# Spreading in one piece, values in four pieces per pair of heads, and scores begun one half tile ahead

## The chip, the cores and the metric

The kernel runs on one core of one Trainium2 chip. The metric is the device time of one launch in microseconds (us). The engines are PE (matrix products), DVE (vector), ACT (scalar functions and copies), POOL (GpSimd) and SP, which here only starts transfers.

## The reference, cut to what matters

Four batches of eight heads, 576 positions, 64 wide; then two layers of 2304 tokens.

```python
def _attn_ref(q, k, v, tau):
    scores = q.shape[-1] ** -0.5 * np.matmul(q, k.transpose(0, 1, 3, 2))
    thresh = np.max(scores, axis=-1, keepdims=True) - tau
    scores = np.where(scores >= thresh, scores, -1000000000.0)
    attn = np.exp(scores - np.max(scores, axis=-1, keepdims=True))
    attn = attn / (np.sum(attn, axis=-1, keepdims=True) + 1e-09)
    return np.matmul(attn, v)
# x: (2304, 512) from the heads; w_in (512, 2048), w_out (2048, 512)
h = x @ w_in;  x = (h * np.tanh(softplus(h))) @ w_out       # layer 1
h = x @ w_in2; x = (h * np.clip(h + 3, 0, 6) / 6) @ w_out2  # layer 2
```

## The kernel before, in words

Attention comes first, then the two layers. Both layers split their products into blocks (seven products in place of eight) and each product into high and low parts; that code is untouched but for the rounding of late weights.

Attention takes heads in pairs. A pair has nine tiles of 128 queries (4.5 per head; the tile in the middle holds the last 64 queries of one head and of the other). Eight iterations of two pairs, 18 tiles each, make 144 tiles. I call the tile's number in its pair i (0 to 8), and a step is what an engine does for one tile.

In a step PE computes the scores of tile t in two halves, each with a high and a low part of k, into one of three pairs of PSUM banks (line 590). A half may be 256 or 320 keys wide. Then it does a piece of the previous pair's work, if one is due: the spreading of the reciprocal sums over the partitions (L626) or the products of values (L648, and L657 for the 64 keys left over, the tail). Last it turns tile t-2: for odd i and for i = 8 first the tail (L601), then the four main blocks (L606). The turned tail lies in the last 128 columns of a pair of score banks, so the second half of a tile's scores waits until ACT has copied out the tail that was there (`tail_kept`); the first half waits only for `probs_ready`.

DVE takes the maximum of tile t (L1061), weighs tile t-1 (L1045: probabilities and their sum), and computes the threshold of tile t (L1072). At i = 0 it computes totals and reciprocals of the pair that has just ended (L1077, L1079); at i = 1 and 6 it scales a part of the mixed values (L1052).

ACT, in order: the copy of the spread sums at i = 2 and 3 (L837), the turned tail (L825), the exponential (L844), the turned main blocks (L818). Behind some steps it rounds k of heads 2 and 3 (steps 3 and 5 of the 18, L802), weights for the layers in four parts (steps 15, 16, 17 and 1, L857), and in the last two iterations x (L873).

POOL splits q and k of the next heads, mixes and splits weights. Its copy of the low part of k waits for ACT's rounding. SP's order of transfers is the same before and after; only counts that it waits for differ.

Each engine's order is the written one: an instruction that waits holds up all behind it on its engine.

The numbers of the pieces are in two tables, which say at which i which groups of keys are multiplied (0 to 3 main, 4 tail), for the lower and the upper part of the queries:

```python
part0 = {4: (0,), 5: (1, 2), 6: (3, 4)}
part1 = {7: (0, 1), 8: (2,), 0: (3,), 1: (4,)}
```

## Time and profile before

| | us |
|---|---|
| time of three runs | 1042.05, 1040.82, 1039.70 |
| median | 1040.82 |
| the profiled execution, time | 1039.75 |
| the profiled execution, span in the trace | 1037.8 |
| PE busy | 1017.1 (98%) |
| DVE busy | 864.2 (83%) |
| ACT busy | 639.7 (62%) |
| POOL busy | 548.1 (53%) |

The time is that of the launch, the span what the engines' records cover; 1.95 us lie around it. The granted TensorE clock is 1.0 of full speed (2.4 GHz) in every stretch. Matmuls overlap in the records, and their ends are modelled: the time that a matmul takes up is the distance from its start to the next one's, not its duration. A product of plain fp32 operands has two records for one instruction, so eight records of L626 are four instructions.

### The profile page before, as it was taken

Reading aid. Unit: us, or ns where it says so; the run is one execution under the profiler, and the core shown is the slowest. Engines: PE = TensorE matmul, PEld = TensorE weight load, DVE = VectorE, ACT = ScalarE, POOL = GpSimd, SP = SyncE. Lnnn points to the kernel's source line nnn. Section 1 sums busy time; section 2 is a strip of 40 time slices with the busy share of each in tenths; the row PEclk is TensorE's granted clock in tenths of the full one; section 3 lists DMA queues with packets and bytes.
Section 4 is the critical chain, followed back from the end, with each engine's and each line's share of the span. In section 5 each row is a group of like instructions: output and inputs, shape, how many; then the busy total and the mean of one; then the engine's idle time right before and its main releaser. Section 6 shows DMA issues by size and latency. Waiting matters only on the chain.

```text
span 1037.8 us, 20190 instructions
## 1 busy us (share of the span) xinstructions
PE 1017.1 (98%) x6984; PEld 928.0 (89%) x6984; DVE 864.2 (83%) x1712; ACT 639.7 (62%) x1209; POOL 548.1 (53%) x578
## 2 busy tenths in 40 slices
PE   5999999999999999999999999999999999999998
PEld 4777777777778999999999999999999999999998
DVE  7888888888875999789997999867996779967884
ACT  5767777778874566455665566555564556555543
POOL 6898898899974830278005750178003850078200
PEclk9999999999999999999999999999999999999999
DMA  6375466467434889589894889643795447753674
GB/s 184 113 218 178 141 214 193 142 205 211 137 113 167 279 298 366 179 269 312 285 392 147 273 303 344 227 147 130 254 310 178 145 170 279 258 172 108 223 244 162
DMA packets 137571, 224.92 MB, mean 217 GB/s; under 512 B 9728, under 2 KB 77824, under 8 KB 137472
## 3 DMA queue, kind: packets, MB, share of 16 engines
q1 hardware_dynamic: 137472, 223.65, 64.8%
q8 instruction: 56, 0.92, 0.4%
q14 instruction: 43, 0.35, 0.1%
HBM read 173.02 MB, written 50.59 MB: 215 GB/s over the span
## 4 chain that ended last, share of the span: by engine, by line
PE 72%; DVE 13%; ACT 6%; issue 5%; DMA 1%; DVEq 0%; ACTq 0%
PE banks L590 7%; PE banks L648 7%; PE banks L606 6%; PE banks L760 6%; PE banks L759 6%; PE banks L758 6%; PE banks L766 5%; PE banks L767 5%; PE banks L768 5%; PE banks L723 5%; PE banks L725 5%; PE banks L724 5%; ACT relu L921 3%; PE banks L657 2%; DVE first_kept L1121 2%
## 5 line engine op out<-in xcount | busy, mean ns | idle before, releaser
L1386 POOL TENSOR_TENSOR ring<-raw,ring 128x256 fp32r<-128x256 f32 x336 | 280.6, 871 | 385.0 <-ACT ring L886 385.0
L723 PE MATMUL banks<-x_high,ring 128*128 128x384 f32 x672 | 228.0, 339 | 3.9 <-ACT first_kept L898 1.7
L725 PE MATMUL banks<-x_high,ring 128*128 128x384 f32 x672 | 225.0, 335 | 0.0
L724 PE MATMUL banks<-x_low,ring 128*128 128x384 f32 x672 | 224.9, 335 | 0.0
L759 PE MATMUL banks<-ring,g_high 128*128 128x256 f32 x504 | 142.6, 283 | 0.0
L760 PE MATMUL banks<-ring,g_low 128*128 128x256 f32 x504 | 142.6, 283 | 0.0
L758 PE MATMUL banks<-ring,g_high 128*128 128x256 f32 x504 | 142.6, 283 | 0.0
L1061 DVE TENSOR_REDUCE neg_max<-banks 128x1 f32<-128x576 f32 x144 | 107.8, 749 | 41.0 <-PE banks L590 38.8
L723 PEld LDWEIGHTS banks<-x_high,ring 128*128 128x128 f32 x672 | 126.1, 188 | 14.2 <-issue 9.4
L724 PEld LDWEIGHTS banks<-x_low,ring 128*128 128x128 f32 x672 | 126.2, 188 | 0.0
L725 PEld LDWEIGHTS banks<-x_high,ring 128*128 128x128 f32 x672 | 126.2, 188 | 0.0
L844 ACT ACTIVATE exps<-banks,neg_max 128x576 f32<-128x576 f32 x144 | 108.1, 751 | 21.8 <-DVE neg_max L1061 21.0
L1045 DVE SCALAR_TENSOR_TENSOR probs<-banks,thresh,exps 128x576 f32<-128x576 f32 x144 | 116.4, 808 | 0.2 <-ACT exps L844 0.2
L766 PE MATMUL banks<-g_high,ring 128*128 128x384 f32 x336 | 112.3, 334 | 0.3 <-DMA ring<-w_out_mix 0.3
L768 PE MATMUL banks<-g_low,ring 128*128 128x384 f32 x336 | 112.2, 334 | 0.0
L767 PE MATMUL banks<-g_high,ring 128*128 128x384 f32 x336 | 112.2, 334 | 0.0
L590 PE MATMUL banks<-k_high,q_stack 128*128 128x256 f32 (+1 forms) x320 | 102.0, 335 | 7.6 <-DVE k_low L1036 7.6
L760 PEld LDWEIGHTS banks<-ring,g_low 128*128 128x128 f32 x504 | 96.7, 192 | 0.0
L759 PEld LDWEIGHTS banks<-ring,g_high 128*128 128x128 f32 x504 | 96.7, 192 | 0.0
L758 PEld LDWEIGHTS banks<-ring,g_high 128*128 128x128 f32 x504 | 96.7, 192 | 0.0
L606 PE MATMUL banks<-ident,probs 128*128 128x128 f32 x576 | 89.7, 278 | 3.8 <-ACT probsT L818 2.9
L936 ACT CAST g_high<-g_rest 128x384 fp32r<-128x384 f32 x120 | 61.6, 514 | 49.3 <-PE banks L760 26.7
(104 smaller groups left out, 2245.4 us busy)
## 6 DMA issues: line engine op xcount, KB each, us to landing
ring<-w_out_mix SPq DMA_DIRECT2D x168, 512.0 KB, 5.1
raw<-w_in_mix SPq DMA_DIRECT2D x48, 896.0 KB, 5.8
w_in_mix<-prep_in SPq DMA_DIRECT2D x18, 896.0 KB, 4.9
w_out_mix<-prep_high SPq DMA_DIRECT2D x16, 896.0 KB, 4.4
w_out_mix<-prep_low SPq DMA_DIRECT2D x16, 896.0 KB, 6.5
q_raw<-qT SPq DMA_DIRECT2D x64, 144.0 KB, 2.9
k_raw<-kT SPq DMA_DIRECT2D x64, 144.0 KB, 3.0
prep_in<-w_in SPq DMA_DIRECT2D x64, 128.0 KB, 3.1
```

Of the source, the lines that this page charges most:

```text
L590: mm = nc.tensor.matmul(bank_pair(s)[:, begin:begin + last - first], lhs, rhs[:, first:last], start=(n == 0), stop=(n == len(products) - 1))
L606: mm = nc.tensor.transpose(turned[:, P * j:P * j + P], own[:, first + P * j:first + P * j + P], ident[:, :])
L723: nc.tensor.matmul(dst, w[:, 0, cols], high, start=(t == 0 and m < 4), stop=False, skip_group_check=True)
L724: nc.tensor.matmul(dst, w[:, 0, cols], low, start=False, stop=False, skip_group_check=True)
L725: mm = nc.tensor.matmul(dst, w[:, 1, cols], high, start=False, stop=(t == KH - 1), skip_group_check=True)
L758: nc.tensor.matmul(to, high[:, rows], w[:, 0, :], start=begin and t % 2 == 0, stop=False, skip_group_check=True)
L759: nc.tensor.matmul(to, high[:, rows], w[:, 1, :], start=False, stop=False, skip_group_check=True)
L760: mm = nc.tensor.matmul(to, low[:, rows], w[:, 0, :], start=False, stop=end, skip_group_check=True)
L766: nc.tensor.matmul(dst[:, d, :], w[:, 0, cols], high, start=begin, stop=False, skip_group_check=True)
L767: nc.tensor.matmul(dst[:, d, :], w[:, 1, cols], high, start=False, stop=False, skip_group_check=True)
L768: mm = nc.tensor.matmul(dst[:, d, :], w[:, 0, cols], low, start=False, stop=end, skip_group_check=True)
L1386: nc.gpsimd.tensor_tensor(ring_slot(slot)[:, 1, :], raw[q % 2][:, m, :], f32(ring_slot(slot)[:, 0, :]), ALU.subtract).then_inc(w_low_ready, 1)
```

## The change

Five things are changed.

First, the pieces. The spreading is done at i = 2 in one piece (its 64 tail columns go to a score bank, the 512 main ones to bank 7), and ACT copies it in two instructions one behind the other. Values come at i = 4 (key groups 0, 1, 2), 6 (3, 4), 8 (0, 1, 2 of the upper part) and 0 (3, 4). So steps 1, 3, 5 and 7 have no piece.

Second, the order on PE. In an odd step PE computes both halves of tile t and the first half of tile t+1, then turns tile t-2; in the even step that follows it starts with the second half. Which tiles have their tail turned in one transpose with their neighbour is numbered anew; the number of transposes stays.

Third, DVE: odd steps take the maximum and the threshold only, even steps weigh tile t-1 and then tile t at once. At i = 0 the totals come between the maximum and the threshold of tile 0, and only tile 0 is left to weigh. The scaling of the lower part moves from i = 6 to i = 7.

Fourth, ACT: in even steps the exponential comes first. k is rounded at steps 4 and 6 in place of 3 and 5. Weights are rounded in three parts at steps 17, 0 and 1, and those that are prepared during the layers in two parts in place of four, on ACT and on DVE.

Fifth, behind the last tile the remaining pieces of attention and the first seven products of the layer are written out in a new order with fewer changes between them.

The core of the diff:

```diff
     def tail_first(i):
-        return i % 2 == 1
-    def turns_tail(i):
-        return tail_first(i) or i == PAIR_TILES - 1
+        return i % 2 == 1 or i == PAIR_TILES - 1
     def tail_rows(i):
-        return UPPER if turns_tail(i) else LOWER
+        return UPPER if i % 2 == 1 else LOWER
...
+        SPREAD_AT = 2
+        MIX0_AT = {4: (0, 1, 2), 6: (3, 4)}
+        MIX1_AT = {8: (0, 1, 2), 0: (3, 4)}
...
+        spread_main = banks[:, 7, 0:MAIN * P]
+        def spread_tail(pair):
+            bank = 1 if pair < PAIRS - 1 else 5
+            return banks[:, bank, BANK - P:BANK - P + TAIL]
...
-        PREP_PARTS = (slice(0, 2), slice(2, 4), slice(4, 6), slice(6, MIXES))
+        PREP_PARTS = (slice(0, 3), slice(3, 5), slice(5, MIXES))
+        LATE_PARTS = (slice(0, 4), slice(4, MIXES))
+        def parts_of(unit):
+            return PREP_PARTS if unit < QUADS - 1 else LATE_PARTS
...
+                if half == 0:
+                    if i in (0, MAIN):
+                        pe.wait_ge(q_low_ready[2 * p + i // MAIN], it + 1)
+                        pe.wait_ge(k_low_ready[2 * p + i // MAIN], it + 1)
+                    after(pe, probs_ready, t - 2)
+                else:
+                    after(pe, tail_kept, tails_turned(max(t - 2, 0)))
+                    if i == SPREAD_AT + 1:
+                        after(pe, spread_kept, 2 * (it * PAIRS_IT + p) - 1)
...
-            part0 = {4: (0,), 5: (1, 2), 6: (3, 4)}
-            part1 = {7: (0, 1), 8: (2,), 0: (3,), 1: (4,)}
-            def attention_step(it, s, ahead=True):
+            def attention_step(it, s):
                 t, p, i = it * TILES_IT + s, s // PAIR_TILES, s % PAIR_TILES
-                first = isinstance(it, int) and it == 0
-                if ahead:
-                    score_tile(it, s)
                 pair, b = it * PAIRS_IT + p - 1, (p + 1) % 2
-                if not first or p == 1:
-                    if i in (2, 3):
-                        spread_sums(pair, b, i - 2)
-                    if i in part0:
-                        mix(it, pair, b, 0, part0[i])
-                    if i in (7, 8):
-                        mix(it, pair, b, 1, part1[i])
-                if not first and i in (0, 1):
-                    mix(it, pair - 1, 1 - b, 1, part1[i])
-                if (not first or s >= 2) and (ahead or s < 2):
+                if even(i):
+                    if i == 0:
+                        score_half(it, s, 0)
+                    score_half(it, s, 1)
+                    if i == SPREAD_AT and pair >= 0:
+                        spread_sums(pair, b, t)
+                    if i in MIX0_AT and pair >= 0:
+                        mix(it, pair, b, 0, MIX0_AT[i])
+                    if i == 8 and pair >= 0:
+                        mix(it, pair, b, 1, MIX1_AT[i])
+                    if i == 0 and pair >= 1:
+                        mix(it, pair - 1, 1 - b, 1, MIX1_AT[i])
+                else:
+                    score_half(it, s, 0)
+                    score_half(it, s, 1)
+                    score_half(it, s + 1, 0)
...
+            last, b = PAIRS - 1, (PAIRS - 1) % 2
+            end = ITS * TILES_IT
+            pe.wait_ge(tail_kept, tails_turned(end - 2))
+            up(0, 0, A11_B11)
+            up(0, 0, S1_T1)
+            mix(ITS, last - 1, 1 - b, 1, MIX1_AT[0])
+            turn(end - 2, TILES_IT - 2)
+            pe.wait_ge(tail_kept, tails_turned(end - 1))
+            up(0, 0, S2_T2)
+            up(0, 0, S3_T3)
+            turn(end - 1, TILES_IT - 1)
+            pe.wait_ge(tail_kept, tails_turned(end))
+            spread_sums(last, b, end + 1)
+            up(0, 0, A12_B21)
+            mix(ITS, last, b, 0, range(MAIN + 1))
+            up(0, 0, S4_B22)
+            mix(ITS, last, b, 1, range(MAIN + 1))
+            up(0, 0, A22_T4)
...
+            def keep_spread(pair):
+                act.wait_ge(spread_ready, pair + 1)
+                nc.scalar.copy(spread[:, MAIN * P:SEQ], spread_tail(pair)).then_inc(spread_kept, 1)
+                nc.scalar.copy(spread[:, 0:MAIN * P], spread_main).then_inc(spread_kept, 1)
+            def take_exp(t, s):
+                act.wait_ge(max_ready, t + 1)
+                after(act, probs_ready, t - 1)
+                nc.scalar.activation(exps[:, s % 2, :], scores_of(s), ACT.Exp,
+                                     bias=neg_max[:, s % 3:s % 3 + 1], scale=1.0).then_inc(exp_ready, 1)
+            rounds = {4: 2, 6: 3}
+            def attention_step(it, s):
                 t, p, i = it * TILES_IT + s, s // PAIR_TILES, s % PAIR_TILES
-                first = isinstance(it, int) and it == 0
-                if i in (2, 3) and (not first or p == 1):
-                    u, pair = i - 2, it * PAIRS_IT + p - 1
-                    act.wait_ge(spread_ready, 2 * pair + u + 1)
-                    nc.scalar.copy(spread[:, PART_AT[u]:PART_AT[u + 1]], mixed[u]).then_inc(spread_kept, 1)
-                if (not first or s >= 2) and (ahead or s < 2):
-                    keep_tail(t - 2, (s - 2) % TILES_IT)
-                if ahead:
-                    act.wait_ge(max_ready, t + 1)
-                    after(act, probs_ready, t - 1)
-                    nc.scalar.activation(exps[:, s % 2, :], scores_of(s), ACT.Exp,
-                                         bias=neg_max[:, s % 3:s % 3 + 1], scale=1.0).then_inc(exp_ready, 1)
-                if (not first or s >= 2) and (ahead or s < 2):
-                    keep_main(t - 2, (s - 2) % TILES_IT, it * PAIRS_IT + (s - 2) // PAIR_TILES)
-                if ahead and s in rounds:
+                pair, pair2 = it * PAIRS_IT + p - 1, it * PAIRS_IT + (s - 2) // PAIR_TILES
+                if even(i):
+                    take_exp(t, s)
+                    if i == SPREAD_AT and pair >= 0:
+                        keep_spread(pair)
+                    if t >= 2:
+                        keep_tail(t - 2, (s - 2) % TILES_IT)
+                        keep_main(t - 2, (s - 2) % TILES_IT, pair2)
+                else:
+                    if t >= 2:
+                        keep_tail(t - 2, (s - 2) % TILES_IT)
+                    take_exp(t, s)
+                    if t >= 2:
+                        keep_main(t - 2, (s - 2) % TILES_IT, pair2)
+                if s in rounds:
...
-                    if s in (15, 16, 17) and it < ITS - 1:
-                        round_prep(0, it, s - 15)
-                    if s == 1 and it > 0:
-                        round_prep(0, it - 1, 3)
+                    if s == 17 and it < ITS - 1:
+                        round_prep(0, it, 0)
+                    if s < 2 and it > 0:
+                        round_prep(0, it - 1, 1 + s)
...
-                after(dve, main_turned, t - 1)
+                after(dve, main_turned, t - 1 if i == 1 else t - 2)
...
                                         mixed[u], spread[:, PART_AT[u]:PART_AT[u + 1]], ALU.mult).then_inc(x_ready, 1)
-            def attention_step(it, s, ahead=True):
+            def take_recips(pair, b):
+                dve.wait_ge(probs_ready, (pair + 1) * PAIR_TILES)
+                nc.vector.tensor_scalar(totals[:, b, :], sums[:, b, :], 1e-9, None, ALU.add).then_inc(totals_ready, 1)
+                dve.wait_ge(totals_ready, pair + 1)
+                nc.vector.reciprocal(recips[:, b, :], totals[:, b, :]).then_inc(recips_ready, 1)
+            def attention_step(it, s):
                 t, p, i = it * TILES_IT + s, s // PAIR_TILES, s % PAIR_TILES
-                first = isinstance(it, int) and it == 0
-                if ahead:
-                    dve.wait_ge(scores_ready, t + 1)
-                    nc.vector.tensor_reduce(neg_max[:, s % 3:s % 3 + 1], scores_of(s), AX_X, ALU.max,
-                                            negate=True).then_inc(max_ready, 1)
                 pair, b = it * PAIRS_IT + p - 1, (p + 1) % 2
-                if i == 6 and (not first or p == 1):
+                if i == 7 and pair >= 0:
                     scale_mixed(pair, 0)
-                if i == 1 and not first:
+                if i == 1 and pair >= 1:
                     scale_mixed(pair - 1, 1)
-                if (not first or s >= 1) and (ahead or s < 1):
-                    weigh(t - 1, (s - 1) % TILES_IT)
-                if ahead:
-                    dve.wait_ge(max_ready, t + 1)
-                    nc.vector.tensor_scalar(thresh[:, s % 3:s % 3 + 1], neg_max[:, s % 3:s % 3 + 1], -1.0, tau_abs[:, :],
-                                            ALU.mult, ALU.subtract).then_inc(thresh_ready, 1)
-                if i == 0 and (not first or p == 1) and (ahead or s == 0):
-                    dve.wait_ge(probs_ready, (pair + 1) * PAIR_TILES)
-                    nc.vector.tensor_scalar(totals[:, b, :], sums[:, b, :], 1e-9, None, ALU.add).then_inc(totals_ready, 1)
-                    dve.wait_ge(totals_ready, pair + 1)
-                    nc.vector.reciprocal(recips[:, b, :], totals[:, b, :]).then_inc(recips_ready, 1)
+                dve.wait_ge(scores_ready, t + 1)
+                nc.vector.tensor_reduce(neg_max[:, s % 3:s % 3 + 1], scores_of(s), AX_X, ALU.max,
+                                        negate=True).then_inc(max_ready, 1)
+                if i == 0 and pair >= 0:
+                    take_recips(pair, b)
+                elif even(i) and i > 0:
+                    weigh(t - 1, s - 1)
+                dve.wait_ge(max_ready, t + 1)
+                nc.vector.tensor_scalar(thresh[:, s % 3:s % 3 + 1], neg_max[:, s % 3:s % 3 + 1], -1.0, tau_abs[:, :],
+                                        ALU.mult, ALU.subtract).then_inc(thresh_ready, 1)
+                if even(i):
+                    weigh(t, s)
...
```

How the orders differ, at three places. PE, step 5 of a first pair and the start of step 6, before (`k_high_85`, `k_low_86`: head 1; L648: values of the previous pair; L601 and L606: the turn of tile 3, L601 its tail):

```order
L590 MATMUL banks<-k_high_85,q_stack_84 128x320 [waits probs_ready]
L590 MATMUL banks<-k_low_86,q_stack_84 128x320
L590 MATMUL banks<-k_high_85,q_stack_84 128x256 [waits tail_kept]
L590 MATMUL banks<-k_low_86,q_stack_84 128x256
L648 MATMUL banks<-probsT_80,values 64x256 x4
L601 MATMUL banks<-ident,probs 128x128 [waits probs_ready]
L606 MATMUL banks<-ident,probs 128x128 [waits main_kept]
L606 MATMUL banks<-ident,probs 128x128 x3
L590 MATMUL banks<-k_high_85,q_stack_84 128x256 [waits probs_ready]
L590 MATMUL banks<-k_low_86,q_stack_84 128x256
L590 MATMUL banks<-k_high_85,q_stack_84 128x320 [waits tail_kept]
```

and now (L610 scores, L622 and L627 the turn):

```order
L610 MATMUL banks<-k_high_78,q_stack_77 128x320 [waits probs_ready]
L610 MATMUL banks<-k_low_79,q_stack_77 128x320
L610 MATMUL banks<-k_high_78,q_stack_77 128x256 [waits tail_kept]
L610 MATMUL banks<-k_low_79,q_stack_77 128x256
L610 MATMUL banks<-k_high_78,q_stack_77 128x256 [waits probs_ready]
L610 MATMUL banks<-k_low_79,q_stack_77 128x256
L622 MATMUL banks<-ident,probs 128x128 [waits probs_ready]
L627 MATMUL banks<-ident,probs 128x128 [waits main_kept]
L627 MATMUL banks<-ident,probs 128x128 x3
L610 MATMUL banks<-k_high_78,q_stack_77 128x320 [waits tail_kept]
L610 MATMUL banks<-k_low_79,q_stack_77 128x320
```

The piece between scores and turn is gone, the first half of tile 6 (its 256 keys) has moved up in front of the turn, and what stands right behind the turn is now the half that waits for `tail_kept`, for the very tail whose transpose stands four transposes ahead of it.

ACT, steps 0, 1 and the start of 2, before (L857: rounding of weights):

```order
L825 COPY tailT<-banks 128x128 [waits tail_turned]
L844 ACTIVATE exps<-banks,neg_max 128x576 [waits probs_ready,max_ready]
L818 COPY probsT_89<-banks 128x4x128 [waits main_turned]
L825 COPY tailT<-banks 128x128 [waits tail_turned]
L844 ACTIVATE exps<-banks,neg_max 128x576 [waits probs_ready,max_ready]
L818 COPY probsT_89<-banks 128x4x128 [waits main_turned]
L857 CAST prep_high<-prep_out 128x256 [waits prep_out_stored,prep_out_mixed]
L837 COPY spread<-banks 128x256 [waits spread_ready]
L844 ACTIVATE exps<-banks,neg_max 128x576 [waits probs_ready,max_ready]
```

and now (L901: rounding of weights; L862, L863: copies of the spread sums):

```order
L870 ACTIVATE exps<-banks,neg_max 128x576 [waits probs_ready,max_ready]
L856 COPY tailT<-banks 128x128 [waits tail_turned]
L849 COPY probsT_89<-banks 128x4x128 [waits main_turned]
L901 CAST prep_high<-prep_out 128x512 [waits prep_out_stored,prep_out_mixed]
L856 COPY tailT<-banks 128x128 [waits tail_turned]
L870 ACTIVATE exps<-banks,neg_max 128x576 [waits probs_ready,max_ready]
L849 COPY probsT_89<-banks 128x4x128 [waits main_turned]
L901 CAST prep_high<-prep_out 128x512 [waits prep_out_stored,prep_out_mixed]
L870 ACTIVATE exps<-banks,neg_max 128x576 [waits probs_ready,max_ready]
```

Two roundings (of 512 each) stand here now where one of 256 stood, one in front of the tail copy of step 1 and one in front of the exponential of step 2; those of steps 15 and 16 are gone.

DVE, two steps, before and now (L1045 and L1090 weigh, L1061 and L1116 take the maximum, L1072 and L1123 compute the threshold):

```order
L1061 TENSOR_REDUCE neg_max<-banks 128x1 [waits scores_ready]
L1045 SCALAR_TENSOR_TENSOR probs,sums<-banks,thresh,exps 128x576 [waits main_turned,thresh_ready,exp_ready]
L1072 TENSOR_SCALAR thresh<-neg_max,tau_abs 128x1 [waits max_ready]
L1061 TENSOR_REDUCE neg_max<-banks 128x1 [waits scores_ready]
L1045 SCALAR_TENSOR_TENSOR probs,sums<-banks,thresh,exps 128x576 [waits main_turned,thresh_ready,exp_ready]
L1072 TENSOR_SCALAR thresh<-neg_max,tau_abs 128x1 [waits max_ready]
```

```order
L1116 TENSOR_REDUCE neg_max<-banks 128x1 [waits scores_ready]
L1123 TENSOR_SCALAR thresh<-neg_max,tau_abs 128x1 [waits max_ready]
L1116 TENSOR_REDUCE neg_max<-banks 128x1 [waits scores_ready]
L1090 SCALAR_TENSOR_TENSOR probs,sums<-banks,thresh,exps 128x576 [waits main_turned,thresh_ready,exp_ready]
L1123 TENSOR_SCALAR thresh<-neg_max,tau_abs 128x1 [waits max_ready]
L1090 SCALAR_TENSOR_TENSOR probs,sums<-banks,thresh,exps 128x576 [waits main_turned,thresh_ready,exp_ready]
```

The second weighing follows the maximum of its own tile with one weighing and one threshold between them; before, a whole step lay between.

## Rows read from the trace of the kernel before

**Rows 1.** Windows: attention, layers. Busy PE, PEld, DVE, ACT, POOL; clock, DMA share, GB/s.
```profile
24.50:304.50 280.00, 278.48 (x2273) 206.38 (x2271) 235.85 (x596) 211.87 (x422) 249.85 (x222) 1.00 0.56 174
324.70:1037.80 713.10, 706.30 (x4496) 696.62 (x4494) 604.50 (x1054) 404.57 (x747) 270.88 (x322) 1.00 0.70 238
```

**Rows 2.** Waits in 100 to 200 us: who waited for whom, total, times, longest.
```profile
ACT tailT L825 <- PE banks L601: 17.3, 21, 1.4
```

**Rows 3.** PE timeline, first pair. Start, duration, engine, line, names, shape, count.
```profile
15.10 0.31 PE L590 MATMUL banks<-k_low,q_stack 128*128 128x320 f32 x1
15.25 0.60 PE L606 MATMUL banks<-ident,probs 128*128 128x128 f32 x4
15.60 0.39 PE L590 MATMUL banks<-k_high,q_stack 128*128 128x320 f32 x1
```

**Rows 4.** PE timeline, last tile of a pair with a values piece.
```profile
171.19 0.31 PE L590 MATMUL banks<-k_low,q_stack 128*128 128x320 f32 x1
171.43 0.76 PE L648 MATMUL banks<-probsT,values 128*64 128x320 f32 x4
172.12 0.66 PE L606 MATMUL banks<-ident,probs 128*128 128x128 f32 x4
172.53 0.36 PE L590 MATMUL banks<-k_high,q_stack 128*128 128x256 f32 x1
```

**Rows 5.** PE timeline, end of attention (bracket: idle before, releaser).
```profile
305.58 0.41 PE L723 MATMUL banks<-x_high,ring 128*128 128x384 f32 x1 [0.81 <-issue]
...
308.54 0.33 PE L601 MATMUL banks<-ident,probs 128*128 128x128 f32 x1
...
309.23 0.44 PE L723 MATMUL banks<-x_high,ring 128*128 128x384 f32 x1
...
314.58 0.77 PE L626 MATMUL banks<-ident,recips 128*64 128x128 f32 x12 [0.70 <-ACT spread L837]
...
320.16 1.83 PE L648 MATMUL banks<-probsT,values 128*64 128x320 f32 x12
```

**Rows 6.** ACT timeline, the copy of the tail between two of those.
```profile
308.91 0.27 ACT L825 COPY tailT<-banks 128x128 f32<-128x128 f32 x1 [0.86 <-PE banks L601]
```

**Rows 7.** PE timeline, first spreading piece of a pair.
```profile
177.36 0.66 PE L626 MATMUL banks<-ident,recips 128*64 128x128 f32 x8
178.20 0.63 PE L606 MATMUL banks<-ident,probs 128*128 128x128 f32 x4 [0.18 <-ACT probsT L818]
```

**Rows 8.** ACT timeline, main copy, rounding of k, exponential.
```profile
166.74 0.59 ACT L818 COPY probsT<-banks 128x512 f32<-128x512 f32 x1
167.20 0.69 ACT L802 CAST k_high<-k_raw 128x576 fp32r<-128x576 f32 x1
167.78 0.76 ACT L844 ACTIVATE exps<-banks,neg_max 128x576 f32<-128x576 f32 x1
```

**Rows 9.** ACT timeline, a rounding of x in the last iteration.
```profile
273.92 0.85 ACT L873 CAST x_high<-x_mix 128x768 fp32r<-128x768 f32 x1
```

**Rows 10.** DVE timeline, totals of a pair, three pairs in a row.
```profile
137.28 1.06 DVE L1077 TENSOR_SCALAR totals<-sums 128x9 f32<-128x9 f32 x1
...
156.17 0.41 DVE L1077 TENSOR_SCALAR totals<-sums 128x9 f32<-128x9 f32 x1
...
174.89 1.06 DVE L1077 TENSOR_SCALAR totals<-sums 128x9 f32<-128x9 f32 x1
```

**Rows 11.** POOL timeline, the operation beside the first of them.
```profile
137.16 1.15 POOL L1327 TENSOR_TENSOR q_stack<-q_raw,q_scale 128x576 fp32r<-128x576 f32 x1
```

**Rows 12.** DVE timeline, a reduce that waits, then two weighings.
```profile
162.97 0.76 DVE L1061 TENSOR_REDUCE neg_max<-banks 128x1 f32<-128x576 f32 x1 [0.84 <-PE banks L590]
...
178.64 0.81 DVE L1045 SCALAR_TENSOR_TENSOR probs<-banks,thresh,exps 128x576 f32<-128x576 f32 x1
...
180.17 0.81 DVE L1045 SCALAR_TENSOR_TENSOR probs<-banks,thresh,exps 128x576 f32<-128x576 f32 x1
```

**Rows 13.** ACT timeline, the exponential behind the reduce of 162.97 us.
```profile
163.77 0.75 ACT L844 ACTIVATE exps<-banks,neg_max 128x576 f32<-128x576 f32 x1 [0.26 <-DVE neg_max L1061]
```

97 lines of the change are left out of this document (42 added, 55 removed).

## The prediction, made before the changed kernel ran

> **What bounds the kernel now.** I read the page first. PE is busy 98% of the span, but ends of matmuls are modelled, so that share proves little. I then cut the span by stages [rows 1]. From 24.5 to 304.5 us, attention, PE shows 278.5 of 280 us, DVE 236, ACT 212, POOL 250; the clock is 1.00. From 324.7 us on, the layers, PE shows 706.3 of 713.1 us. The change touches attention almost alone, so the question is what sets the 280 us.
>
> The waits give it: ACT stood 17.3 us in 100 for the turned tail [rows 2], and DVE stands for scores (0.84 us before the maximum of 162.97 us, [rows 12]), while DVE needs 1.53 us from one weighing to the next where nothing holds it (178.64 to 180.17 us, [rows 12]): 13.8 us for nine tiles. The totals of three successive pairs start at 137.28, 156.17 and 174.89 us [rows 10]: two pairs take 37.61 us, so a pair takes 18.8. PE sets it: DVE and ACT stand for PE in most steps, PE hardly ever for them. What PE saves counts in full, and what makes PE wait costs in full.
>
> Next I looked at how PE's time is spent when it changes the kind of its products. In the first pair no piece of older work is due: the last score product starts at 15.10, the first transpose at 15.25, the next scores at 15.60 us [rows 3]. 0.15 us is what a product of 320 columns takes, so this change costs nothing, and four transposes take 0.35 us. With a piece of values between, the last score product starts at 171.19, the piece at 171.43 (0.24: 0.09 more), the transposes at 172.12 and the next scores at 172.53 us (0.41: 0.06 more) [rows 4]. The four records of the piece take 0.69 us. Twelve such records last 1.83 and four 0.76 us [rows 5, 4], so four more cost 0.54 us, and 0.15 us of the 0.69 is fixed. A piece costs 0.09 + 0.15 + 0.06 = 0.30 us beside its products.
>
> The Trainium skill says it too ("TensorEngine Tiling (Array Packing)", Key Properties): changing the tiling mode drains the engine. The pieces write 64 columns of the array (128*64 in the rows), scores and transposes 128. The trace agrees, at 0.30 us for the way there and back. What the rule alone would make of the change is a rival below.
>
> **The change, part by part.** The sum is made against the profiled execution, 1039.75 us (span 1037.8 and 1.95 around it); it lies 1.07 us under the median of the three runs, 1040.82, and I add the sum to the median.
>
> (a) *Fewer pieces.* Before, each of nine steps has one, now five (i = 0, 2, 4, 6, 8). The products are the same ones. Four fewer, at 0.30 us, are -1.20 us in each of the 15 pairs in which pieces are done: -18.0 us. In the steps with a tail, where the 0.06 us may not show, it may be 0.23 us: -13.8 us.
>
> (b) *The tail's hand-over.* In an odd step PE now turns tail and main blocks of tile t-2 and then starts the second half of tile t+1, which waits until ACT has copied that tail. Before, the first half stood between and hid it. The end of attention shows the price: tail transpose 308.54, ACT's copy 308.91, the waiting product 309.23 us [rows 5, 6], 0.69 us from transpose to product, with 0.16 us of it a wait by the weight loads. Without the wait PE would need 0.09 (one transpose, a quarter of 0.35) + 0.35 = 0.44 us. So each hand-over costs 0.25 us; if the first transpose still takes 0.17 as at the end, 0.17 us, and then (a) is the smaller one. All four odd steps have a tail: +1.00 us a pair, +15.0 us in 15; bounds +10.2 and, if ACT is busy at that moment, more (d, f). Queued behind the waiting half are the piece and the turn of the even step; DVE's maximum waits for it.
>
> (c) *The old wait at i = 2.* The first spreading piece has eight records from 177.36 us, and the transposes start at 178.20, of which 0.18 us is a wait for ACT's main copy [rows 7]; in the other pair of an iteration I see none with that label. I take 0.13 us a pair as gone, -2.0 us (0 to -2.7). Nothing is late next there: the totals and sums are ready two steps earlier.
>
> So (a) to (c) are -5.0 us: the large saving is handed back almost whole by (b).
>
> (d) *ACT's roundings.* After a turn ACT makes the main copy, then at steps 4 and 6 the rounding of k, then the next tail copy. Copy at 166.74, rounding 167.20, next at 167.78 us [rows 8]: 1.04 us, and 0.3 us before it (as between the tail's transpose and its copy, 0.37) make 1.34. Meanwhile PE does six score products (0.86 us by the distances of rows 3: about 0.13 each and 0.08 for the first) and its tail transpose; its copy could start 0.37 later, at 1.23. So each costs 0.1 us. The weights' parts in steps 0 and 1 each hold up something: the second, in front of the exponential of tile 2 and so of the spread sums' copy, by about 0.2 us. Together 0.4 us an iteration, in 7: +2.8 us. Lower end 0; upper end the whole of one rounding (0.69) and as much for a weights' part, 1.4 an iteration: +9.8. POOL gets the rounded k some 2.5 us later in an iteration and has had waits of that size for it, so it costs nothing until that grows.
>
> (e) *Totals.* They now stand between the maximum of tile 0 and its weighing. They last 1.06 or 0.41 us [rows 10]: the one at 137.28 ends at 138.34, and POOL's operation beside it runs from 137.16 to 138.31 us [rows 11]. The weighing must wait anyway for the exponential: maximum at 162.97, exponential at 163.77, 0.75 long [rows 12, 13], so about 1.58 us from the maximum's start; the other work fits in while the totals take up to 0.6. Excess 0.46 us in one pair of two, half of it reaching PE: +0.2 us an iteration, +1.4 us. Bounds: 0, and 1.15 us (the POOL operation) in each of 15 pairs if all reached PE, +17.
>
> The Trainium skill ("SBUF — State Buffer", Who interferes with whom) says that a tensor_scalar of DVE may take the port pair shared with GpSimd and that the second to ask is blocked until the first is done. The trace agrees (both ends within 0.03 us); by the rule the price would be 0 to one POOL operation in each pair, with the new phase unknown, which is what the bounds above say.
>
> (f) *x in the last two iterations.* Roundings of x, 0.85 us long [rows 9], follow steps 2, 4, 6 of the last iteration and step 10 of the one before. Behind a k rounding that is already late, one costs nearly its full length: 0.7 + 0.7 us, 0.5 at step 2, 0.3 before: +2.2 us (0 to +3.4).
>
> (g) *The end.* Seven pieces become four, -0.9 us; the wait of 0.70 us between the two spreading pieces at 314.58 [rows 5] is gone; one more hand-over shows, +0.16; the first product of the layer waited 0.81 us for its weights [rows 5] and will wait about 0.15 less, as the piece of step 8 is longer. -1.6 us (-2.4 to 0: the single spreading also waits for two copies, behind which the values stand).
>
> (h) *The start.* Tile 1's maximum now waits for tile 0's weighing: one maximum, 0.76 us, at most, made up in the pair that has no pieces: +0.3 us. The late roundings in two parts save two starts each on DVE and ACT, nine times, in a stage where PE is full [rows 1]: -0.3 us (-2 to +0.5, the upper if DVE waits for ACT's longer first part).
>
> Sum: -5.0 + 2.8 + 1.4 + 2.2 - 1.6 + 0.3 - 0.3 = -0.2 us. Forecast: no change, 1040.7 us, where 0.2% (2.1 us) is about what a measurement can tell from none.
>
> **The rivals.**
>
> *ACT and DVE cannot keep the chain between them (slower).* PE now has ACT's tail copy in its path four times a pair, and behind each turn ACT has main copy, rounding and tail copy in a row. It decides when the copy starts later than 0.37 us after its transpose: every 0.1 us there, in four steps and 15 pairs, is 6 us. With (d) at 1.0 us an iteration (+4.2 more than the sum), and (e) at 0.4 (+1.4 more): 1040.6 + 5.6 = 1046.2 us. For it: ACT has no slack at steps 4 and 6 by my count. Against: it was idle 17.3 us in 100 [rows 2].
>
> *The side costs are covered (faster).* If (d), (e) and (f) fall where something else waits, 6.4 us of the sum go: 1034.3 us. For it: in even steps the piece of values leaves ACT and DVE over 1 us. Against: PE is the bound, so there is little else to hide behind.
>
> *The tail is no hand-over at all (much faster).* (a), (c) and (g) stay and (b) is nothing: 1040.8 - 18.0 - 2.0 - 1.6 + 6.4 = 1025.6 us. That needs ACT's copy to be there 0.44 us after the transpose; the rows show 0.69 [rows 5, 6]. It is also what the Trainium skill's rule on modes ("TensorEngine Tiling (Array Packing)", Key Properties) would give if nothing else counted.
>
> *It doesn't do what it says: DVE becomes the bound.* In a pair of steps the two weighings are tied to the second maximum: about 1.3 us from maximum to maximum (PE's pace) and 2.4 from there to the next maximum, 3.7 four times, 2.7 at i = 0 and 0.8 of scaling: 18.3 us a pair, against PE's 18.5. So near that pair times of 18.8 may stay as they are: 1041 us, the forecast's time for another reason.
>
> **How the numbers follow.** Forecast case, with the last rival, 0.40, of which four fifths lie within 2.1 us. Slower case 0.27. Faster case 0.28. Much faster 0.05. Its own range is 1037 to 1044; as cases of both signs hold more than half, the stated one reaches into both: 1033 (the faster case with (b) a little cheap) to 1047 (the slower one), which leaves out the much faster case and the ends of (e). Faster by over 0.2%: 0.28 + 0.05 + 0.03 = 0.36. Within: 0.33. Slower: 0.27 + 0.04 = 0.31.
>
> **What would show it.** (a) From the last score product to the first transpose of a step without a piece: 0.15 us or less. (b) From a tail transpose in an odd step to the second half of the next scores: 0.69 us, and PE or its loads waiting for the tail copy about 60 times. Pairs of 18.4 us where ACT rounds nothing, 18.8 to 19.0 where it does. (d) The tail copy at steps 5 and 7 of a first pair starts 0.1 us later than in a second pair. (e) Totals whose end is that of a POOL operation. (g) No wait of 0.70 us for the copy of spread sums at the end. I am wrong if the half behind the turn doesn't wait, or if a pair takes over 19 us in the middle of attention.

## The result, and the profile after

The changed kernel takes 1048.55 us (median of 4 runs, 1048.01 to 1050.06), the one before 1041.14 on the same chip (4 runs); the ratio is 1.0074 (95% interval 1.0059 to 1.0089). It is slower by some 7.4 us. The forecast was no change, 1040.7 us, with 1033 to 1047 as its range; the measured time lies 1.5 us above it.

The windows of the profile after, as in [rows 1]: attention from the same start, in a window 20 us longer, then the layers from their second quad on (a quad is one of the groups in which a layer's upward products are done, seven products each; busy time of PE, its weight loads, DVE, ACT, POOL; clock, DMA share, GB/s).

```profile
24.50:324.50 300.00, 282.98 (x2293) 217.59 (x2293) 244.72 (x606) 223.42 (x422) 252.16 (x219) 0.98 0.53 163
340.40:1044.90 704.50, 702.01 (x4496) 697.28 (x4494) 597.23 (x1037) 402.69 (x729) 272.81 (x322) 1.00 0.70 240
```

Two things moved, in opposite directions. The second quad starts at 340.4 us where it started at 324.7: attention and its end cost 15.7 us more. From there to the end of the last product it is 702.7 us, where it was 709.7 (1043.1 - 340.4 and 1034.4 - 324.7): 7 us less. Together +8.7 us, the difference of the spans. In attention PE is busy for 283 of 300 us, where it was for 278.5 of 280 [rows 1].

What took its time is in the waits of 24.5 to 304.5 us (who waited for whom: us, times, longest; PEld, the weight loads, and PE often wait for the same thing at once, so their lines aren't added).

```profile
POOL k_low L1387 <- ACT k_high L833: 33.1, 7, 7.7
ACT tailT L856 <- PE banks L622: 13.6, 48, 0.5
PEld banks L664 <- DMA values_tail<-v: 12.6, 6, 3.9
PE banks L664 <- DMA values_tail<-v: 11.0, 6, 3.7
PEld banks L610 <- ACT tailT L856: 10.3, 31, 1.4
PE banks L610 <- ACT tailT L856: 2.9, 4, 1.1
```

The hand-over that I had forecast is there (L610 for the tail), but in front of it stands a wait that no line of the prediction names: PE waits for a pair's values six times, 11.0 us. All six waits are in the step of tile 4 in the first pair of an iteration. The PE timeline in the fourth iteration (start, duration, engine, line, names, shape, count, idle before):

```profile
170.03 0.31 PE L610 MATMUL banks<-k_high,q_stack 128*128 128x320 f32 x1
170.18 0.31 PE L610 MATMUL banks<-k_low,q_stack 128*128 128x320 f32 x1
173.25 2.83 PE L664 MATMUL banks<-probsT,values 128*64 128x256 f32 x12 [2.76 <-DMA values_tail<-v]
176.01 1.12 PE L627 MATMUL banks<-ident,probs 128*128 128x128 f32 x4
176.78 0.61 PE L610 MATMUL banks<-k_high,q_stack 128*128 128x320 f32 x1
```

Twelve products of values last 2.83 us here, and 1.51 us after one of the shorter waits; the transposes last 1.12 and 0.66. The clock tells why (windows with the granted clock third from the right: the stretch of low clock, and 4.4 us ahead of it).

```profile
172.40:179.20 6.80, 5.95 (x27) 4.43 (x28) 1.63 (x4) 1.59 (x4) 0.74 (x1) 0.50 0.11 36
168.00:172.40 4.40, 2.44 (x17) 1.87 (x15) 3.49 (x9) 3.23 (x7) 2.66 (x3) 0.99 0.58 156
```

The clock fell to 0.50 (1.2 GHz) at 172.4 us, in the wait, and stayed there 6.8 us. At 93.8, 0.6 us after the longest wait had ended, it did so for 3.4 us. An estimate: of these 10.2 us the first 0.85 are still part of the wait, and half of the other 9.35 is 4.7 us of lost time; 11.0 + 4.7 = 15.7 us, as much as attention lost.

Who was late? First POOL, then SP's issues (L430 is k_raw of head 3, L440 to L442 the values of the odd pair), and ACT behind PE's wait:

```profile
165.59 1.41 POOL L1387 TENSOR_TENSOR k_low<-k_raw,k_high 128x576 fp32r<-128x576 f32 x1
...
178.46 1.41 POOL L1387 TENSOR_TENSOR k_low<-k_raw,k_high 128x576 fp32r<-128x576 f32 x1 [7.65 <-ACT k_high L833]
```

```profile
167.02 1.10 SPq L430 DMA_DIRECT2D k_raw<-kT  x2
168.17 1.11 SPq L440 DMA_DIRECT2D values<-v  x2
169.32 0.48 SPq L441 DMA_DIRECT2D values_tail<-v  x1
169.84 0.60 SPq L442 DMA_DIRECT2D values_tail<-v  x1
```

```profile
177.16 0.59 ACT L849 COPY probsT<-banks 128x512 f32<-128x512 f32 x1 [5.10 <-PE banks L627]
177.65 0.67 ACT L833 CAST k_high<-k_raw 128x576 fp32r<-128x576 f32 x1
```

It is a ring. SP sends k_raw of head 3 when POOL has done k_low of head 1 (167.0 us), and the values stand behind it in SP's order; they land at about 173.2, 3.4 us after the last of them is issued, and PE could have used them at 170.4. PE's wait holds up its turn, so ACT's copy, so the rounding of k, which the change put behind this very step (177.65); POOL has stood 7.65 us for it, and is late with the next k_low of head 1 an iteration on. In the kernel before the same issue of the last values came at 159.40 us and PE's piece at 162.87, 3.5 us later: there was no slack to give away, and I had not looked.

What was forecast within a pair is there too. An odd step (PE timeline; L622 turns the tail, L610 of 147.21 is the half that waits for ACT's copy of it):

```profile
146.47 0.28 PE L610 MATMUL banks<-k_low,q_stack 128*128 128x256 f32 x1
146.58 0.27 PE L622 MATMUL banks<-ident,probs 128*128 128x128 f32 x1
146.69 0.63 PE L627 MATMUL banks<-ident,probs 128*128 128x128 f32 x4
147.21 0.41 PE L610 MATMUL banks<-k_high,q_stack 128*128 128x320 f32 x1
```

The turn follows the scores by 0.11 us (no piece between, as in [rows 3]) and the half waits 0.17 us: 0.63 from tail to product, where 0.11 + 0.35 would do. The second pair of an iteration takes 18.25 us (from the maximum of its tile 0 to that of the next pair's), where it was 18.89. I call it the odd pair, and the first one, in which ACT rounds k, the even pair; that one was 18.71. In the odd steps 1, 5 and 7 of an even pair the same distance from tail to product is mostly 0.75 to 0.81 us.

### The profile page after: what moved, and what is told of

Same layout as the page of the kernel before. It is cut to its first block, busy times and chain, and to the rows that moved or that the text cites. A ratio compares the mean times of both kernels' runs of the same rounds, so it can differ in the third digit from the quotient of the medians.

```text
span 1046.5 us, 20128 instructions
## 1 busy us (share of the span) xinstructions
PE 1012.6 (97%) x6984; PEld 937.2 (90%) x6984; DVE 861.9 (82%) x1694; ACT 645.3 (62%) x1184; POOL 548.7 (52%) x571
## 4 chain that ended last, share of the span: by engine, by line
PE 60%; POOL 13%; DVE 6%; ACT 5%; issue 5%; DMA 3%; SPq 3%; DVEq 0%; POOLq 0%; ACTq 0%
PE banks L741 7%; PE banks L743 7%; PE banks L742 7%; PE banks L778 6%; PE banks L777 6%; PE banks L776 6%; PE banks L785 6%; PE banks L784 6%; PE banks L786 6%; ACT relu L965 3%; POOL prep_low L1410 2%; PE banks L664 2%; POOL q_stack L1379 2%; POOL k_low L1387 2%; POOL prep_in L1396 2%
## 5 line engine op out<-in xcount | busy, mean ns | idle before, releaser
L1116 DVE TENSOR_REDUCE neg_max<-banks 128x1 f32<-128x576 f32 x144 | 108.6, 754 | 41.0 <-PE banks L610 40.4
L1090 DVE SCALAR_TENSOR_TENSOR probs<-banks,thresh,exps 128x576 f32<-128x576 f32 x144 | 117.1, 813 | 14.5 <-ACT exps L870 10.5
L610 PE MATMUL banks<-k_high,q_stack 128*128 128x320 f32 (+1 forms) x320 | 105.4, 345 | 14.2 <-DVE k_low L1080 7.9
L849 ACT COPY probsT<-banks 128x512 f32<-128x512 f32 x144 | 84.6, 588 | 32.9 <-PE banks L627 31.1
L627 PE MATMUL banks<-ident,probs 128*128 128x128 f32 x576 | 92.5, 284 | 3.9 <-ACT probsT L849 3.2
```

What stands on the lines that cost most here:

```text
L1090: nc.vector.scalar_tensor_tensor(out=probs_of(t), in0=scores_of(s), scalar=thresh[:, s % 3:s % 3 + 1], in1=exps[:, s % 2, :], op0=ALU.is_g ...
L1116: nc.vector.tensor_reduce(neg_max[:, s % 3:s % 3 + 1], scores_of(s), AX_X, ALU.max, negate=True).then_inc(max_ready, 1)
```

## The experiments

The first four runs: the ring, and the layers. Ratios are to the kernel before, with their 95% interval; it took 1041.56, 1040.61 and 1040.94 us beside the three groups of runs, which were made on three chips, so small differences between runs are safer by the ratios.

**Values earlier.**

```
                 store_prep_in(0, it - 1)
+                if it > 1:
+                    load_values(it - 1, 1)
                 load_head(it, 3)
-                if it > 1:
-                    load_values(it - 1, 1)
```

> The changed kernel, with the values of the odd pair put in front of head 3 in SyncE's order instead of behind it. Theory (the values come late because their transfer stands behind k_raw of head 3, which waits for GpSimd's k_low of head 1, and GpSimd has been made late by the moved rounding of k): the six waits of 3.7 us for values and values_tail go, and with them the low clock behind each. The iterations, of 38.6 to 42.4 us now, come to two pairs of 18.2 to 18.4 us, and the time to 1024 to 1031 us. Rival (transfers are late whatever their order, since the shorter iteration is less than GpSimd's and SyncE's work for it): the wait moves to the q or k of a head, and the time stays within 1042 to 1049. Rival (the hand-over of the tail to ScalarE is what costs): no more than 2 us change.

1034.58 us, 0.9932 (0.9920 to 0.9944): 14 us less than the changed kernel. No wait for values is left, and the clock is 1.00. The last values of the odd pair are now issued at 154.92 us, and PE's piece follows the scores at once:

```profile
154.92 0.61 SPq L442 DMA_DIRECT2D values_tail<-v  x1
```

```profile
164.51 0.31 PE L610 MATMUL banks<-k_low,q_stack 128*128 128x320 f32 x1
164.75 1.52 PE L664 MATMUL banks<-probsT,values 128*64 128x256 f32 x12
```

The place of the values' transfers in SP's order is worth the whole loss. The time stayed 3.6 us over the top of what I had expected: an iteration takes 37.2 to 37.7 us, and the last two 38.4 and 40.2 (the last one up to the first product of the layers; 37.6 and 38.2 in the kernel before).

**k at 3 and 5.**

```
-            rounds = {4: 2, 6: 3}
+            rounds = {3: 2, 5: 3}
```

> The changed kernel, with ScalarE's rounding of k back behind steps 3 and 5. Theory (the late rounding starts the ring ScalarE, GpSimd, SyncE, values, TensorE): GpSimd is done some 2.5 us sooner, the waits for the values shrink from 3.7 us to 1 us or less, and the time comes to 1028 to 1038 us. Rival (the values come late because the pairs have become shorter, not because k is rounded later): the waits stay near 3.7 us, and the time within 1045 to 1049. In either case a k cast now stands in an odd step, where GpSimd gets it sooner and the tail's hand-over may grow by 0.5 us at two steps of 18.

1033.82 us, 0.9928 (0.9916 to 0.9940). One wait for the values is left, 0.6 us. So the ring can be cut at either place.

**The late k alone, in the kernel before.** The same line, the other way round: `rounds = {4: 2, 6: 3}`.

> The kernel before, with only ScalarE's rounding of k moved from behind steps 3 and 5 to behind steps 4 and 6. Theory (the values had no slack, and this move alone makes them late): a wait for values_tail appears on TensorE, some 2 us at the middle of most iterations, and the time is 1045 to 1056 us. Rival (with pairs of 18.8 us there is room for the move): 1040 to 1042 us.

1047.95 us, 1.0064 (1.0051 to 1.0078): this line alone makes the kernel before slower by 6.4 us. The waits of its attention:

```profile
POOL k_low L1339 <- ACT k_high L802: 23.0, 7, 5.5
ACT prep_high L857 <- POOL prep_out L1356: 10.8, 6, 2.1
PEld banks L648 <- DMA values_tail<-v: 3.7, 6, 1.4
PE banks L590 <- ACT tailT L825: 3.5, 6, 0.8
PE banks L648 <- DMA values_tail<-v: 1.9, 4, 1.1
```

An iteration takes 38.2 to 38.8 us instead of 37.6. POOL is late for the rounded k here too, but it reaches PE on two paths. The values are one, 1.9 us. The larger is another, 3.5 us: POOL's mixed weights (`prep_out`) come late, ACT stands for them in front of their rounding, and PE for the tail that ACT copies behind it (ACT, then PE; in the kernel before ACT's waits for `prep_out` are 1.4 us and PE has none for the tail):

```profile
155.65 0.62 ACT L857 CAST prep_high<-prep_out 128x512 fp32r<-128x512 f32 x1 [1.83 <-POOL prep_out L1356]
```

```profile
156.49 0.42 PE L590 MATMUL banks<-k_high,q_stack 128*128 128x320 f32 x1 [0.61 <-ACT tailT L825]
```

So my theory of this run had the time right and only part of the cause; the same edit together with earlier values, which would tell the two paths apart, was not run. The changed kernel has moved these roundings to other steps and shows no such wait of ACT. The values' waits are shorter here (1.1 at most) and the clock stays up; in the changed kernel the loss is twice as large. The rival, that shorter pairs alone made the values late, falls with k at 3 and 5.

**The late rounding alone, in the kernel before.** Two parts for the units of the layers, four as ever in attention:

```
+        LATE_PARTS = (slice(0, 4), slice(4, MIXES))
-                mixes = PREP_PARTS[n]
+                mixes = parts_of(unit)[n]
```

> The kernel before, with only the late rounding in two pieces in place of four (attention stage as before). The layers of the changed kernel are 7 us shorter in the traces. Theory (the two pieces give all of it): 1034 to 1036 us, attention unchanged at 324.7 us. Rival (the two pieces give the 0.3 us of the sum in the prediction, and the 7 us come from another part of the change or from the clock): 1040 to 1041.5 us.

1036.06 us, 0.9943 (0.9928 to 0.9958): 5.5 us less, for an edit that I had put at 0.3. Attention was not unchanged in this trace: its last exponential starts at 308.0 us, before at 304.6, though nothing in that stage's work was edited; in the control below it starts at 304.4. No cause is shown for these 3.4 us. From the last exponential to the end of the span it is 726.1 us, before 733.2: 7.1 us less.

**The late rounding undone, in the changed kernel.** `LATE_PARTS` as four slices.

> The changed kernel with only the late rounding put back to four pieces. If the late rounding gives in the changed kernel what it gives in the kernel before (5.5 us by the medians of e3_before_two_late, 7 us by the traces): 1054 to 1056 us. Rival (in the changed kernel the layers are shorter for another reason): 1048 to 1050 us.

1056.52 us, 1.0153 (1.0139 to 1.0167), 8 us more than the changed kernel (0.79% by the ratios), a little over the first theory. Both ways round, the two parts are worth 5.5 to 8 us by the times, and 7.1 and 7.2 us by the distance from the last exponential to the end (731.9 us here, 724.7 in the changed kernel). The groups of DVE's low parts, in the layers of the kernel before and then of the changed one (busy us, mean ns; idle before):

```profile
L1200 DVE TENSOR_TENSOR prep_low<-prep_out,prep_high 128x512 fp32r<-128x512 f32 x27 | 26.6, 1036 | 0.0
L1200 DVE TENSOR_TENSOR prep_low<-prep_out,prep_high 128x256 fp32r<-128x256 f32 x9 | 6.4, 715 | 0.0
```

```profile
L1248 DVE TENSOR_TENSOR prep_low<-prep_out,prep_high 128x1024 fp32r<-128x1024 f32 x9 | 12.7, 1417 | 1.2 <-ACT prep_high L901 1.2
L1248 DVE TENSOR_TENSOR prep_low<-prep_out,prep_high 128x768 fp32r<-128x768 f32 x9 | 11.8, 1310 | 0.0
```

18 pieces less save 8.5 us of DVE for the same columns, 0.47 us for each. The traces show when a piece has this price: when POOL runs beside it. The four pieces of a unit in the kernel before, first with POOL busy all the time, then with POOL idle (no POOL record from 381.0 to 383.7 us):

```profile
353.15 5.38 POOL L1386 TENSOR_TENSOR ring<-raw,ring 128x256 fp32r<-128x256 f32 x5
353.59 4.34 DVE L1200 TENSOR_TENSOR prep_low<-prep_out,prep_high 128x512 fp32r<-128x512 f32 x4
381.24 2.23 DVE L1200 TENSOR_TENSOR prep_low<-prep_out,prep_high 128x512 fp32r<-128x512 f32 x4
```

With two pieces it is 2.68 and 3.17 us beside POOL, 2.09 without it (at 369.82, 346.32 and 395.85 us of the changed kernel's trace). POOL makes the low parts of the weights that PE waits for. The waits of PE and of its weight loads in the layers, before:

```profile
PEld banks L723 <- issue: 7.7, 22, 0.8
PEld banks L723 <- POOL ring L1386: 2.8, 4, 0.9
PE banks L723 <- ACT first_kept L898: 1.7, 3, 0.6
PE banks L723 <- DVE first_kept L1121: 0.9, 3, 0.5
```

and after:

```profile
PEld banks L741 <- issue: 3.8, 12, 0.5
PE banks L741 <- DVE first_kept L1169: 0.6, 3, 0.2
```

The lines of PEld and PE overlap (the loads' wait of 0.85 us that ends at 359.43 and PE's of 0.56 at 359.46 are one). PEld's alone are 10.5 us before and 3.8 after, 6.7 less, about what the layers gained. They follow the edit in both kernels: 3.5 us with the two parts in the kernel before, 10.6 with the four in the changed one. Busy, PE shows 706.3 of 713.1 us before [rows 1]; these waits were in that "full" stage. How DVE's pieces reach the weight loads is not shown link by link: most of the waits have no releaser in the profile ("issue").

**One late part.** `LATE_PARTS = (slice(0, MIXES),)`, with both mends of the ring (as the next kernel).

> As e6_both, with the late rounding of the layers in one piece instead of two. Theory (each late piece on VectorE costs some 0.8 us at its start, by 8.7 us for eight of four parts and 5.9 us for four of two, and two pieces have already taken away TensorE's waits for the weights' low parts): within 1 us of e6_both. Rival (what counts is VectorE's time, wait or no wait): nine pieces fewer at 0.8 us on VectorE, some 3 to 5 us less. Rival (the first piece is now so long that it holds up ScalarE's gates): 2 to 5 us more.

1034.08 us, 0.9929 (0.9916 to 0.9943), against 1033.66 and 0.9934 with two parts: no change. From the last exponential to the end it is 724.6 us, with two parts 724.8, and the weight loads' waits are 3.6 us. DVE has 5.3 us less to do (19.2 against 24.5 us in these pieces), and it gives nothing: what counted was PE's waits, and two parts have taken those that can be taken this way.

**Both mends**, and as its control the kernel before with two late parts and the values earlier.

> The changed kernel with both mends: the values of the odd pair in front of head 3 in SyncE's order, and k rounded behind steps 3 and 5. Theory (each mend alone removes the same wait, and what is left is other): no wait for values, iterations of 37.2 to 37.4 us as with each alone, and 1032.5 to 1034.5 us. Rival (the two remove different losses: with the values earlier the odd pairs took 18.25 us, with k earlier the even pairs 18.8 us, and together an iteration takes 37.05 us): 1030.5 to 1032 us.

1033.66 us, 0.9934 (0.9922 to 0.9945): the first theory, one wait removed by either mend. Iterations take 37.3 to 37.4 us, and the last two 37.6 and 38.0.

> The kernel before with the late rounding in two pieces and the values of the odd pair in front of head 3: the control. Theory (with pairs of 18.8 us the values arrive just in time, so an earlier order has nothing to give): as e3_before_two_late, 1034 to 1037 us. Rival (an earlier transfer also frees GpSimd or SyncE for what follows): 1031 to 1033 us. The distance to e6_both is what the change's attention part is worth without the late values.

1032.97 us, 0.9932 (0.9919 to 0.9944). That is the top of the rival's range, but its interval overlaps both that of the late parts alone and that of both mends, so whether the earlier values give anything here stays open. So the change's attention part, freed of the ring, is worth nothing that can be measured, as the sum of the prediction had it. Both mends put k back behind steps 3 and 5; the run with the values earlier alone keeps it where the change put it, and lies 1.6 us above this control by the times and level with it by the ratios (0.9932 both).

**A sixth piece.** Both mends, and key 2 in a piece of its own behind the turn of tile 4's step.

```
-        MIX0_AT = {4: (0, 1, 2), 6: (3, 4)}
+        MIX0_AT = {4: (0, 1), 6: (3, 4)}
...
+                if i == 4 and pair >= 0:
+                    mix(it, pair, b, 0, (2,))
```

> As e6_both, but the values' piece of step 4 is cut in two, with the turn between (keys 0 and 1 before it, key 2 behind it): one more piece of 64-column products in each pair, the same products in all. It measures the price of a piece. By the prediction's 0.30 us: 15 pairs, 4.5 us more than e6_both. By the rows of the changed kernel (last score to mix 0.09 us, mix to turn 0.07, the turn behind it 0.05): about 0.2 us, 3 us more. Rival (TensorE has time to spare in this step, and a piece is paid by waits): 0 to 1 us more.

1040.02 us, 6.4 us more: 0.42 us in each of 15 pairs, above the 0.30 of the prediction. The piece itself costs 0.34 us in every pair (from the maximum of tile 4 to that of tile 5 2.91 us, with both mends alone 2.57). An odd pair wins as much back by shorter totals. Of the even ones three take 19.1 us, 0.35 more than with both mends, and three 20.0: these three are the ones whose totals last 1.36 to 1.38 us. So the rest of the 6.4 us is totals that fell beside other operations of POOL, and not the price of a piece.

**No half ahead.** Both mends; both halves of a tile's scores stand together in every step.

```
-                    if i == 0:
-                        score_half(it, s, 0)
+                    score_half(it, s, 0)
                     score_half(it, s, 1)
...
-                    score_half(it, s + 1, 0)
```

> As e6_both, but TensorE no longer begins the next tile's scores ahead of a turn: both halves of a tile stand together in every step, and the even step's first half covers the hand-over of the tail. If the hand-over is a cost of the size in the prediction (0.25 us at four places in a pair), it goes: 15 pairs by 1.0 us, 1019 to 1023 us by that price, 1029 to 1032 by the 0.15 us that the rows of the changed kernel show in every second pair. Rival (the half in front of the turn lets VectorE start its maximum 0.46 us sooner, and VectorE waits for scores as often as TensorE for the tail): it costs more than it gives, 1034 to 1040 us.

1042.09 us, 8.4 us more, above the rival's range. The hand-over is gone, and PE waits at the turns instead (attention of this run, then of both mends):

```profile
PEld banks L627 <- ACT probsT L846: 20.2, 58, 0.5
PE banks L627 <- ACT probsT L846: 7.7, 27, 1.2
```

```profile
PEld banks L610 <- ACT tailT L856: 5.7, 20, 1.0
PE banks L627 <- ACT probsT L849: 3.2, 6, 1.5
```

There is one bank for turned blocks; the half in front of the turn covers ACT's main copy out of it. DVE's waits for scores, my rival's reason, rose only from 19.6 to 23.6 us: its direction was right, its mechanism at most a part. Part of the 8.4 us is again the totals, which last 1.02 to 1.08 us in most even pairs here: such pairs take 19.7 to 19.8 us, the two with short ones 19.2, with both mends 18.8.

**Totals.** Once without the instruction, once made by ACT; both with both mends.

```
-                nc.vector.tensor_scalar(totals[:, b, :], sums[:, b, :], 1e-9, None, ALU.add).then_inc(totals_ready, 1)
-                dve.wait_ge(totals_ready, pair + 1)
-                nc.vector.reciprocal(recips[:, b, :], totals[:, b, :]).then_inc(recips_ready, 1)
+                nc.vector.reciprocal(recips[:, b, :], sums[:, b, :]).then_inc(recips_ready, 1)
```

> As e6_both, but the instruction that adds 1e-9 to a pair's sums is left out and the reciprocal reads the sums themselves (the 1e-9 is missing from the result). In e6_both this instruction of 9 columns lasts 0.99 us at 212.82 us, until GpSimd's operation beside it ends, and stands in front of the first weighing; an odd pair takes 18.57 us with it, 18.25 where it happened to be short. Theory (it holds up TensorE through the first weighing): 0.3 to 0.5 us in each of 15 pairs, 5 to 8 us less than e6_both. Rival (the wait only moves to the reciprocal, which asks for the same port): no change. Rival (VectorE has time to spare there): no change, and the reciprocal short.

1030.93 us, 0.9902 (0.9888 to 0.9916): 2.7 us less, half of the 5 to 8 that I had expected. Only the odd pairs in the middle have the long totals, and they go from 18.57 to 18.17 us. The reciprocal doesn't take it over (DVE, attention):

```profile
L1104 DVE RECIPROCAL recips<-sums 128x9 f32<-128x9 f32 x15 | 3.1, 204 | 0.0
```

And on ACT, ahead of the first exponential of a pair:

```
+                nc.scalar.activation(totals[:, b, :], sums[:, b, :], ACT.Identity, bias=tiny[:, :],
+                                     scale=1.0).then_inc(totals_ready, 1)
```

> As e6_both, with the pair's totals (sums plus 1e-9) made by ScalarE ahead of the first exponential, where it waits 0.8 us for VectorE, instead of by VectorE. If the totals on VectorE cost 0.3 to 0.5 us a pair: 1026 to 1029 us. If VectorE now stands for ScalarE's totals, or the port wait moves to the reciprocal: 1032 to 1036 us.

1032.32 us, 0.9919 (0.9906 to 0.9933). 1.3 us under both mends, and the intervals overlap: inconclusive by the times. The trace says more: an iteration takes 37.0 us, as without the totals (36.95), where it takes 37.3 to 37.4 with both mends, and 0.9 us of this are lost again in the first pair, which has a stretch of low clock in this execution (18.06 us, with both mends 17.12). It is the fastest that computes everything, with the control 0.7 us behind and not distinguishable from it.

## Why the prediction was wrong, point by point

The step that failed is the last sentence of (d): "POOL gets the rounded k some 2.5 us later in an iteration and has had waits of that size for it, so it costs nothing until that grows". A wait on an engine that has slack was taken for a wait that nothing hangs on. What hung on it in the changed kernel was SP's queue: k_raw of head 3 waits for POOL's k_low of head 1, and the values stand behind it. Measured: 14 to 15 us by either mend, the waits themselves and the low clock behind two of them. In the kernel before the same line alone costs 6.4 us, there by the values and, more of it, by POOL's late weights. The mechanism was absent from sum, bounds and rivals alike.

(h), the late rounding in two parts, was mis-sized: -0.3 (-2 at best), measured -5.5 and -8. I reasoned that in a stage where PE is full nothing on DVE can matter; the waits of that stage were never read. The share of busy time hid 10.5 us of waits of the weight loads.

The rest of the sum, +0.1 us in the forecast, came out near it: +0.7 us (both mends against their control, each known to some 1.5 us), in part because errors cancelled, which is luck:

- (a) The pieces. From one record's start to the next, in an odd pair, what leads into the pieces of values and sums or stands there in their place (1.67 us, before 2.03), and the pieces with their exits (6.92, before 7.60 without the wait of (c)), take 1.04 us less than before; forecast -1.20, the smaller bound -0.92. The sixth piece costs 0.34 by itself.
- (b) The hand-over: 0.63 us from tail to product in odd pairs, 0.17 over the 0.46 of a turn that doesn't wait. I took 0.25 and had 0.17 as bound: (a) and (b) were both too large, and their errors partly cancelled. PE's loads wait for the tail copy 31 times, not 60.
- (c) The old wait stood in the odd pairs only (0.19 us, in front of the turn at i = 2) and is gone: -1.4 us in all, where I had taken 0.13 us for every pair; where the totals are long, 0.3 to 0.4 us takes its place.
- (d) Its own cost, apart from POOL's, was right: with k behind steps 4 and 6 the hand-overs of steps 5 and 7 of an even pair take 0.81 and 0.75 us, with k behind 3 and 5 0.63 (0.30 us an iteration), and that of step 1, behind a part of the weights, 0.76 in both: 0.43 us an iteration, forecast 0.4.
- (e) 2.7 us with both mends, the instruction itself included, where I had 1.4. In the changed kernel itself the totals lasted 0.37 us on average, and its odd pairs took 18.25 us, 0.08 more than without the instruction; it was not taken out there. (By [rows 12, 13] the exponential ends 1.55 us after the maximum's start, not 1.58; it changes nothing.)
- (f) The last two iterations, the last up to the first product of the layers: 38.4 and 40.2 us with the values earlier, where k is rounded as forecast. Over the 37.4 of its others that is 3.8 us; the kernel before has 0.6 of it by the same measure, so 3.2 us, forecast 2.2 with 3.4 as bound. With k at 3 and 5 it is 2.2, with both mends 0.2.
- (g) From the last exponential to the first downward product of the layers (the second product of a layer) 70.9 us, before 73.5. The two late parts alone give 1.2 of these 2.6 us; the 1.4 left answer to the forecast 1.6. The wait of 0.70 us in front of the second spreading [rows 5] is gone.
- (h) The start was too small by far. The first pair, in which no pieces are due, takes 16.7 to 17.2 us in the runs of the new order (18.0 in the two with a low clock there), and 14.6 to 15.7 in the four of the old one: +1.0 to +2.5 us, forecast +0.3. An iteration in the middle gives 0.24 us back (37.36 with both mends, before 37.6). No run tests what slows the first pair.

Of the rivals, the slower one had nearly the time (1046.2) for a reason that was small. ACT's copy starts 0.31 us after the tail's transpose in most odd steps, 0.43 to 0.49 in steps 1, 5 and 7 of an even pair, and late by much (1.2 us) only in two steps of the last iteration, behind roundings of x. The sign named in advance for being wrong did come: pairs took over 19 us in the middle of attention, 19.9 to 24.2, and each of these had the wait for the values (one without it took 19.07). The signs of single steps came as written, a pair of 18.4 us (18.25) and one of 18.8 to 19.0 among them (18.9 to 19.5 with the values earlier).

Adding up against the kernel before: late rounding -5.5 to -8, the ring +14 to +15, all else about 0: +6 to +9.5, measured +7.4. The values' 15.7 us in the trace (11.0 of waits, 4.7 of clock) agree with the two mends within 2 us.

The Trainium skill's rule on the shared port ("SBUF — State Buffer", Who interferes with whom) was weighed only against the totals. The late pieces are where it would have paid: by the rule each piece may wait for one POOL operation, of 0.88 us here on average. The traces agree: four pieces take 3.85 to 4.39 us beside POOL and 2.23 where it is idle. No run took POOL's work away by itself to test it.

## What to carry to other kernels

When a change makes an engine later, follow what that engine releases to the DMA queue and through it: read what stands behind the released transfer in the same queue, and how much time lies between that transfer's landing and its first use. A transfer that lands just in time shows no wait, and the next edit pays for it. And read the waits of every stage that an edit touches, the "full" ones too: 6.7 us of waits that could be had stood in a stage with PE 99% busy. Price an instruction from a place where the neighbours are as busy as they will be.
